# Evening out the first and last block of a fused scan and two feed-forward layers

## The reference

```python
# x, f_logit: (2, 6080, 256)   lower_bound: (256,)
sig = 1.0 / (1.0 + np.exp(-f_logit))
f = lower_bound + (1.0 - lower_bound) * sig
i = 1.0 - f
for t in range(S):                       # S = 6080 steps
    h = f[:, t] * h + i[:, t] * x[:, t]
    y[:, t] = h
x = y.reshape(2 * 6080, 256)
h = np.maximum(x @ w_in1, 0.0)           # w_in1: (256, 2048)
x = h * h @ w_out1                       # w_out1: (2048, 256)
h = x @ w_in2
g = np.where(h > 0.0, h, np.exp(np.minimum(h, 0.0)) - 1.0)
out = g @ w_out2
```

## Time and profile before

| | |
|---|---|
| time, median of 3 runs | 1965.78 us (1965.6 to 1966.9) |
| span of the profiled execution | 1963.6 us, 2.2 us under the median of the runs |
| busy PE / PEld | 1957.7 us (100%) / 1632.4 us (83%) |
| busy DVE / ACT / POOL | 1604.5 (82%) / 1518.6 (77%) / 643.5 us (33%) |
| mean DMA | 143 GB/s |
| mean granted TensorE clock | 1.000 |

### The profile page before, as it was taken

How to read it: one execution, slowest core, us unless ns; L and a number is a source line. 1 busy time by engine, 2 the same in 40 slices (tenths; PEclk the granted TensorE clock), 3 DMA queues, 4 the chain that set the end, 5 groups by cost and what they waited for, 6 DMA issues and landing times.

```text
span 1963.6 us, 27999 instructions
## 1 busy us (share of the span) xinstructions
PE 1957.7 (100%) x8712; PEld 1632.4 (83%) x8712; DVE 1604.5 (82%) x1806; ACT 1518.6 (77%) x1848; POOL 643.5 (33%) x534
## 2 busy tenths in 40 slices
PE   9999999999999999999999999999999999999999
PEld 7888888888888888888888888888888888888888
DVE  7878887888888788888888888888888887866887
ACT  8898877877778777777777877777787777767766
POOL 4666632323223232232322323223232232332311
PEclk9999999999999999999999999999999999999999
DMA  6677453444444445344444444534434443443453
GB/s 196 204 228 227 165 150 106 148 145 127 147 135 125 130 147 146 107 148 136 126 147 142 127 124 144 147 111 150 135 119 148 145 130 113 137 136 118 140 172 112
DMA packets 228679, 281.54 MB, mean 143 GB/s; under 512 B 153857, under 2 KB 164098, under 8 KB 228610
## 3 DMA queue, kind: packets, MB, share of 16 engines
q1 hardware_dynamic: 226688, 280.23, 46.4%
q10 hardware_dynamic: 1922, 0.46, 0.1%
HBM read 248.25 MB, written 32.37 MB: 143 GB/s over the span
## 4 chain that ended last, share of the span: by engine, by line
PE 100%; DVE 0%; DVEq 0%; issue 0%
PE acc L626 53%; PE ring L626 46%; PE ring L663 0%; PE ring L778 0%; PE acc L785 0%; PE acc L663 0%; PE ring L785 0%; DVE o_sb L1719 0%; PE ring L823 0%; DVEq L116 0%; DVE m_sb L1632 0%
## 5 line engine op out<-in xcount | busy, mean ns | idle before, releaser
L626 PE MATMUL acc<-hid_hi,wout 128*128 128x512 f32 (+1 forms) x3072 | 1149.9, 387 | 0.0
L626 PE MATMUL ring<-t_hi,s_w 128*128 128x512 f32 (+1 forms) x2672 | 1027.3, 387 | 0.0
L626 PEld LDWEIGHTS acc<-hid_hi,wout 128*128 128x128 f32 x3072 | 576.8, 188 | 113.4 <-DMA wout<-w_kept 0.2
L626 PE MATMUL acc<-hid_lo,wout 128*128 128x512 f32 (+1 forms) x1536 | 594.7, 387 | 0.0
L626 PEld LDWEIGHTS ring<-t_hi,s_w 128*128 128x128 f32 x2672 | 501.7, 188 | 99.5 <-ACT xb L1182 0.3
L1895 POOL TENSOR_TENSOR xb<-xb,m_sb 128x512 f32<-128x512 f32 (+1 forms) x184 | 236.3, 1284 | 971.4 <-DVE hid_lo L1530 971.4
L626 PE MATMUL ring<-t_lo,s_w 128*128 128x512 f32 (+1 forms) x1336 | 517.2, 387 | 0.0
L1174 ACT ACTIVATE m_sb<-ring 128x512 f32<-128x512 f32 (+1 forms) x184 | 109.2, 593 | 354.1 <-PE ring L626 345.4
L626 PEld LDWEIGHTS acc<-hid_lo,wout 128*128 128x128 f32 x1536 | 288.4, 188 | 56.6
L626 PEld LDWEIGHTS ring<-t_lo,s_w 128*128 128x128 f32 x1336 | 250.9, 188 | 49.6
L1530 DVE TENSOR_TENSOR hid_lo<-xa,hid_hi 128x1024 fp32r<-128x1024 f32 (+1 forms) x191 | 231.3, 1211 | 61.4 <-ACT hid_hi L1153 61.2
(11 more groups left out here) (146 smaller groups left out, 1761.0 us busy)
## 6 DMA issues: line engine op xcount, KB each, us to landing
s_w<-s_kept SPq DMA_DIRECT2D x184, 512.0 KB, 3.8
s_w<-s_kept SPq DMA_DIRECT2D x184, 384.0 KB, 4.0
wout<-w_kept SPq DMA_DIRECT2D x88, 512.0 KB, 4.3
out_dram<-o_sb SPq DMA_DIRECT2D x88, 128.0 KB, 3.6
f_raw<-in_f_logit_dram SPq DMA_DIRECT2D x168, 64.0 KB, 3.5
x_raw<-in_x_dram SPq DMA_DIRECT2D x168, 64.0 KB, 2.7
s_kept<-ee SPq DMA_DIRECT2D x16, 512.0 KB, 4.1
s_kept<-s_w SPq DMA_DIRECT2D x8, 512.0 KB, 4.0
```

The source lines that it names most:

```text
L626: mm = nc.tensor.matmul(out_ap, lhs[a], rhs[b], start=start and t == 0, stop=stop and t == 2)
```

## The change

The first and the last block get 480 steps each; the ten between keep 512. Block i now starts at step 480 + 512 (i - 1). Block 0 is loaded and turned in pieces of 240 steps (`H0`) with 2 rows for each of 120 partitions (`P0`). The end's pieces are of 8 and 7 groups of 32 steps, in place of 7 and 7.

```diff
-    S_TAIL = T - N_FULL * S
+    S_TAIL = (T - (TAIL - 1) * S) // 2
+    H0 = S_TAIL // 2
+    P0 = S_TAIL // 4
     def steps_of(i):
-        return S_TAIL if known(i, TAIL) else S
+        return S_TAIL if known(i, TAIL) or known(i, 0) else S
+
+    def start_of(i):
+        return 0 if known(i, 0) else S_TAIL + i * S - S
...
-        MID = S_TAIL // SQ // 2
-        END_PIECES = ((1, 0, MID), (1, MID, 2 * MID), (0, 0, MID), (0, MID, 2 * MID))
+        KS = S_TAIL // SQ
+        MID = (KS + 1) // 2
+        END_PIECES = ((1, 0, MID), (1, MID, KS), (0, 0, MID), (0, MID, KS))
...
-                o = dst[:, b, half].rearrange("p (k d) -> p k d", d=D)
-                rows = src[b, half * HALF:(half + 1) * HALF, :].rearrange("(p k) d -> p k d", p=P)
+                o = dst[0:P0, b, half].rearrange("p (k d) -> p k d", d=D)
+                rows = src[b, half * H0:(half + 1) * H0, :].rearrange("(p k) d -> p k d", p=P0)
...
-                    rows = out_v[b, bass.ds(n * S, S_), a * ROWRUN:(a + 1) * ROWRUN]
+                    rows = out_v[b, bass.ds(start_of(n), S_), a * ROWRUN:(a + 1) * ROWRUN]
...
-                    mm = triple(o[:, f], [s_w[:, pr.par(), QI[f, c], h, :] for h in range(2)],
-                                [t[v][:, BI[c, n], :] for t in (t_hi, t_lo)], c == 0, c == 1)
+                    mm = triple(o[:, f, 0:pr.N], [s_w[:, pr.par(), QI[f, c], h, :] for h in range(2)],
+                                [t[v][:, BI[c, n], 0:pr.N] for t in (t_hi, t_lo)], c == 0, c == 1)
...
-                rows = src[:, b, h].rearrange("p (k e c) -> p c k e", k=2, c=CH)[:, c]
+                rows = src[0:P0, b, h].rearrange("p (k e c) -> p c k e", k=2, c=CH)[:, c]
                 o = dst.rearrange("p (e k) -> p k e", k=2)
                 for k in range(2):
-                    mm = nc.tensor.transpose(o[:, k], rows[:, k], ident)
+                    mm = nc.tensor.transpose(o[:, k], rows[:, k], ident[0:P0, 0:P0])
```

More of the change, by code:

```diff
@@ L48, in gated_scan_two_ffn @@
     assert HALF < S_TAIL < S and S_TAIL % SQ == 0 and N_FULL >= 4
+    assert (TAIL - 1) * S + 2 * S_TAIL == T
     def known(i, block):
@@ L369, in end_store @@
             for a in parts:
-                rows = out_v[b, TAIL * S + k0 * SQ:TAIL * S + k1 * SQ, a * ROWRUN:(a + 1) * ROWRUN]
+                rows = out_v[b, start_of(TAIL) + k0 * SQ:start_of(TAIL) + k1 * SQ, a * ROWRUN:(a + 1) * ROWRUN]
                 i = o_sb[a * SQ:(a + 1) * SQ, b, k0:k1, :, :]
@@ L662, in up_first @@
                     for f in range(2):
-                        mm = nc.tensor.matmul(o[:, f], s_w[:, pr.par(), QI[f, c], a, :],
-                                              (t_lo if b else t_hi)[0][:, BI[c, n], :],
+                        mm = nc.tensor.matmul(o[:, f, 0:pr.N], s_w[:, pr.par(), QI[f, c], a, :],
+                                              (t_lo if b else t_hi)[0][:, BI[c, n], 0:pr.N],
                                               start=c == 0 and t == 0, stop=c == 1 and t == 2)
@@ L1082, in plain_relu @@
             def plain_relu(pr, n):
-                t = (xa if n else xb)[:, pr.par()]
+                t = (xa if n else xb)[:, pr.par(), :, 0:pr.N]
                 act.wait_ge(up_n1 if n else up_n0, pr.g + 1)
@@ L1089, in plain_relu @@
                     act.wait_ge(lo_n1 if n else lo_n0, pr.g - 1)
-                nc.scalar.activation(t, plain_banks(pr, n), ACT.Relu).then_inc(relu_n1 if n else relu_n0, 1)
+                nc.scalar.activation(t, plain_banks(pr, n)[:, :, 0:pr.N], ACT.Relu).then_inc(relu_n1 if n else relu_n0, 1)
             def plain_square(pr, n):
-                t = (xa if n else xb)[:, pr.par()]
+                t = (xa if n else xb)[:, pr.par(), :, 0:pr.N]
                 act.wait_ge(relu_n1 if n else relu_n0, pr.g + 1)
@@ L1211, in tanh0_first @@
                 act.wait_ge(f0_loaded[1][h], DMA_INC)
-                nc.scalar.activation(xa[:, 1, h], xa[:, 1, h], ACT.Tanh, scale=0.5).then_inc(tanh0_done, 1)
+                nc.scalar.activation(xa[0:P0, 1, h], xa[0:P0, 1, h], ACT.Tanh, scale=0.5).then_inc(tanh0_done, 1)
             def tanh0():
@@ L1217, in tanh0 @@
                     act.wait_ge(f0_loaded[0][h], DMA_INC)
-                nc.scalar.activation(xa[:, 0], xa[:, 0], ACT.Tanh, scale=0.5).then_inc(tanh0_done, 1)
+                nc.scalar.activation(xa[0:P0, 0], xa[0:P0, 0], ACT.Tanh, scale=0.5).then_inc(tanh0_done, 1)
             def gates0_first(h):
@@ L1223, in gates0_first @@
                 act.wait_ge(consts_done, 2)
-                nc.scalar.activation(z_raw[:, 0, 1, h * HALF:(h + 1) * HALF], th_turn[:, 0, HALF:S] if h else th_early,
+                nc.scalar.activation(z_raw[:, 0, 1, h * H0:(h + 1) * H0], th_turn[:, 0, H0:S_TAIL] if h else th_early,
                                      ACT.Identity, scale=amp[:, 0:1], bias=mid[:, 0:1]).then_inc(gates0_done, 1)
@@ L1228, in gates0 @@
                 act.wait_ge(th_turned, place0(b, c))
-                nc.scalar.activation(z_raw[:, c, b, :], th_turn[:, c], ACT.Identity, scale=amp[:, c:c + 1],
+                nc.scalar.activation(z_raw[:, c, b, 0:S_TAIL], th_turn[:, c, 0:S_TAIL], ACT.Identity, scale=amp[:, c:c + 1],
                                      bias=mid[:, c:c + 1]).then_inc(gates0_done, 1)
             def split0_first(h):
-                s = slice(h * HALF, (h + 1) * HALF)
+                s = slice(h * H0, (h + 1) * H0)
                 act.wait_ge(scanned0, h + 1)
@@ L1240, in split0 @@
                 act.wait_ge(scanned0, place0(b, c))
-                nc.scalar.activation(t_hi[0][:, BI[c, b], :], y_raw[:, c, b, :], ACT.Identity,
+                nc.scalar.activation(t_hi[0][:, BI[c, b], 0:S_TAIL], y_raw[:, c, b, 0:S_TAIL], ACT.Identity,
                                      scale=amp[:, c:c + 1]).then_inc(y0_hi, 1)
@@ L1265, in tile0 @@
             def tile0(f, up, relu, acted, hi):
-                t = xb[:, 0, f]
+                t = xb[:, 0, f, 0:S_TAIL]
                 act.wait_ge(up, 1)
-                nc.scalar.activation(t, plain_banks(pr0, 0)[:, f], ACT.Relu).then_inc(relu, 1)
+                nc.scalar.activation(t, plain_banks(pr0, 0)[:, f, 0:S_TAIL], ACT.Relu).then_inc(relu, 1)
                 act.wait_ge(relu, 1)
@@ L1272, in tile0 @@
                 act.wait_ge(acted, 1)
-                nc.scalar.activation(hid_hi[:, 0, 2 + f], t, ACT.Copy).then_inc(hi, 1)
+                nc.scalar.activation(hid_hi[:, 0, 2 + f, 0:S_TAIL], t, ACT.Copy).then_inc(hi, 1)
             act.wait_ge(x0_gated_last, 1)
@@ L1917, in _ @@
                                     channel_multiplier=1).then_inc(ident_done, 1)
-            less = gate.rearrange("p c s -> p (c s)").rearrange("p (k e) -> p k e", e=P)
+            less = gate[0:P0].rearrange("p c s -> p (c s)").rearrange("p (k e) -> p k e", e=P)
             v = rows0(xb, 0)[:, 1]
```

48 lines of the change are left out of this document (24 added, 24 removed).

## The result

| | before | after |
|---|---|---|
| median of the runs | 1965.78 us | 1971.12 us (1970.88 to 1972.1, 7 runs) |
| span of the profiled execution | 1963.6 us | 1969.2 us |
| forecast for after | | 1964.0 us (1962.6 to 1969.2) |

The ratio is 1.0028, with an interval of 1.0018 to 1.0037. So the change costs 5.3 us, 0.28% (0.18% to 0.37%): slower, and outside the range. The granted clock is 0.999 to 1.0 in both, and there are 8712 matmuls in both. One of the seven executions of the kernel before took 4027.16 us; leaving it out moves its median by less than 0.1 us.

The account below looks back on a forecast made before the run. PE was taken to bound the kernel, by matmul count times pace. Pace -2.24, mixed steps 0, opening +0.1, ACT waits +0.3 and end +0.05 gave -1.8 us: 1964.0 us, -0.09%, called no change; range 1962.6 to 1969.2.

Parts of the forecast that it names:

- The bound and the count: Whole kernel: PE bounds the time; matmuls stay at 8712, 768 fewer columns are only 0.32 us, so the pace decides.
- The pace at 480: Matmuls of block 0 and the last block: 213.33 ns each, -9.92 and +7.68 us, together -2.24 us; chance 0.46.
- The rival on the other side: 480-column matmuls run out of step at 216 to 218.3 ns; 1969.0 us at 217; chance 0.30, 0.10 above 217.2.
- The straight line: Rival: 480 columns cost 214.67 ns, on the line through the two measured widths; 1965.9 us; chance 0.14.
- Mixed steps: Steps mixing two widths, 6 before and 12 after: taken as 0, between a gain and a cost of 0.7 us.
- The opening: Start of the kernel, behind scans, gates and splits: +0.1 us, from -0.1 to +0.4.
- The rival of a bad spread: Row transfers for 120 partitions use fewer DMA engines, 3 to 5 us later, 1967 to 1969; chance 0.03.
- Waits where ACT lags: PE waits in the first layers, where ACT carries the weights' splits: +0.3 us, from 0 to +0.8.
- m2's copy: ACT copy PE awaits in the third step of block 0's second layer: wait of 0.1 us forecast to grow +0.2.
- m5's wait: Block 1's first layer, m5 needing m1's copy: slack of 0.4 us forecast to be just used up, +0.1.
- The end: Last activation chain, transposes and store: the wait unchanged, transposes at most 0.05 us more; +0.05.
- the wait that was to stay: PE's wait of 0.18 us before the last pair's first load, behind ACT and DVE; forecast unchanged.

Follow-up runs that it names:

- experiment 1: Matmuls alone, no kernel, each with its own weight load, at widths from 512 to 128: 226.67 ns at 512, 216.67 at 480, 202.67 at 448.
- experiment 6: Changed kernel with block 0 loaded, turned and scanned as 512 steps in 128 partitions, its products still 480: 1970.19 us, ratio 1.0023 to the kernel before.
- experiment 7: Against the kernel before, widths swapped: first block 448 steps in pieces of 112 partitions, last block 512: 1967.42 us, ratio 1.0009.
- experiment 8: First half of the change alone: first block 480, last 448 as before, leaving out each sequence's last 32 steps: 1960.25 us, ratio 0.9972.
- experiments 9 to 11: Changed kernel, 480-column data from column 32 (1971.43 us), 12 (1968.65) or 8 (1972.6); between them TensorE alone in the kernel's order, column 12 at 213.33 ns.
- experiments 7 and 11: 448 first and 512 last, 1967.42 us; and the changed kernel with 480-column data from column 12 and an opening of 512 steps, 1967.28 us.

## Why the prediction was wrong

- **The bound and the count** were right: PE alone bounds the kernel, 8712 matmuls, nearly all of the change in their pace and the opening.
- **The pace at 480: the step that failed.** "By my reason above I take 213.33." It is 216.67. Block 0 and the last block sum to +2.64 us, forecast -2.24: 4.9 of the 7.1 us by which I missed. The reason (a weight load of 188 ns that shows below some 450 columns) is refuted by experiment 1: the extra is 16.67 ns at 480 and 464 as well, and matmuls of 192 columns with their own loads run at 111.5. What the runs show instead: the extra over one column a cycle depends on the width, on the column where the data begins and on the order of the tiles, and without a trend from one width to the next. The two measured widths could not tell it. Worked out from both sides, the bounds (213.33 and 218.3) held it; the choice inside them did not.
- **The rival on the other side** (216 to 218.3 ns, 1969.0 at 217, chance 0.30) holds the measured pace and has its sign right, in part by luck. Its mechanism was a stream that pays for not being of 512; but 496, 416 and 256 columns alone pay 13.33 over one column a cycle as 512 does, and the 5 ns it took its price from are a loss of mixed widths, another effect. Its bounds were also not worked out alike: with its own sum at 217 the limit of 0.2% is reached at 217.5 ns, not 217.2, and the range's upper end of 1969.2 at 217.1, not 217.4. The straight line (214.67) is refuted.
- **Mixed steps: mis-sized.** I took 0 "as 480 is nearer to 512 than 448 is"; it is +1.6. Nearness was no argument: 512 and 480 in threes lose 4.7 ns a matmul, 512 and 448 2.5. My upper end was +0.7.
- **The opening: mis-sized.** +0.1, range to +0.4; it is +1.2, of which experiment 6 gives back 0.96 in the profile (0.75 in the medians). "Fewer bytes can save at most" was the wrong way round: in the stretch of the earlier trace rows loads for 120 partitions move at 251 GB/s where those for 128 move at 354, and alone they take 1.08 to 1.18 times as long. The path was wrong too: the waits were put down to scans and gates, while the last gate waited for its transfer already before. The rival of a bad spread had the right effect, at 0.03, with a price for half the engines; how many engines a load for 120 partitions uses no run here shows.
- **Waits where ACT lags: mis-sized.** +0.3 forecast; the two intervals at m2's copy are 0.18 us over the pace in place of 0.10 before, and m5's wait did not come: +0.1. The slack that I worked out for it did give way at 448 steps (experiment 7). The slower PE at 480 saved less than I had put.
- **The end: mis-sized.** +0.05 forecast, +0.2 measured: the wait that was to stay is gone, and what follows the last matmuls grew by 0.3 where 0.05 was put down. In experiment 8, with 448 last again, it is as long as before.

Measured terms: 2.64 + 1.6 + 1.2 + 0.1 + 0.2 = +5.7 us, against the spans' difference of 5.6. Experiment 8 (1960.25, expected 1960.1) and experiments 9 to 11 test the parts one by one. Not settled is why a pace is what it is: the runs show the dependence, not the mechanism behind it. What switched it at 41 to 42 us in experiments 7 and 11 is known only as far as the late load beside it.

## What to carry to other kernels

A matmul's pace at a width that the trace does not hold is not to be read off its neighbours, however straight the line; measure that width alone, in the kernel's own order of tiles, before a tiling is chosen for it, and keep both bounds' signs open until then. Two widths in turn within a stream can cost more than both alone, so a tiling should have few edges between unequal blocks. A block's length also sets how many partitions its loads fill: fewer rows can cost time where they leave partitions empty, as 120 and 112 did here, while 96 took a little less than 128.

## What the runs showed of the hardware that I had not expected

- float32r matmuls with their own weight loads take 13.33 ns over one column a cycle at 512 and 496 columns, 16.67 at 480 and 464, 16.00 at 448; bfloat16 takes 2.6 at 480.
- Starting the data at another column of the same tile moves the pace by up to 7 ns: 448 columns took 200.0 ns from column 16 and 206.5 to 206.8 from column 8, 480 took 213.3 from 12 and 220.0 from 8 or 24.
- Some places have two steady paces (480 from column 32: 217.8 and 220.0; from 12: 213.3 and 217.8), and a stop of 0.3 us is enough to switch them. In two traces the pace switched where one weight load came 0.1 us late and the matmuls were held by 0.03 us or less.
- The kernel before with its 448 columns read from column 16 took 1964.38 us against 1965.74 in the same batch, 0.9994 (0.9985 to 1.0003). The interval holds no change, but its 11 runs (1964.0 to 1964.9) all lie under the 27 of the kernel before (1965.1 to 1966.4): likely the fastest version here that computes the whole result.
- Four row loads for 120 partitions took 5.9 us twice, for 128 partitions 5.0 and 5.5.
